# The products of the second down-projection, one behind each product of the first block's projections

## The reference

```python
def _attn_ref(q, k, v, tau):                       # q, k, v: 1 x 6016 x 256
    qn = q / (norm(q, axis=1) + 1e-06)
    kn = k / (norm(k, axis=1) + 1e-06)
    s = kn.transpose(0, 2, 1) @ qn / tau           # 256 x 256
    a = softmax(s)
    return v @ a

def _moe_ref(x, w_in, w_out, a, b):                # w_in 256 x 2048, w_out 2048 x 256
    h = x @ w_in
    P = a[0] + a[1] * h + a[2] * h**2 + a[3] * h**3
    Q = 1.0 + abs(b[0]) * abs(h) + abs(b[1]) * h**2
    return (P / (Q + 1e-06)) @ w_out

def _moe2_ref(x, w_in, w_out):
    h = x @ w_in
    return (h * clip(h + 3.0, 0.0, 6.0) / 6.0) @ w_out

out = _moe2_ref(_moe_ref(_attn_ref(q, k, v, tau)))
```

## Time and profile before

| | |
|---|---|
| median of 3 runs | 1137.36 us (1136.55 to 1137.97) |
| profiled execution, own time | 1137.52 us |
| its span | 1135.7 us |
| TensorE busy | 1111.2 us (98%) |
| VectorE, ScalarE, GpSimd busy | 889.9, 878.8, 781.0 us (78%, 77%, 69%) |
| matmuls | 6012 |
| mean granted clock of TensorE | 0.995 |

### The profile page before, as it was taken

How to read it: one execution, slowest core, us unless ns; L and a number is a source line. 1 busy time by engine, 2 the same in 40 slices (tenths; PEclk the granted TensorE clock), 3 DMA queues, 4 the chain that set the end, 5 groups by cost and what they waited for, 6 DMA issues and landing times.

```text
span 1135.7 us, 17913 instructions
## 1 busy us (share of the span) xinstructions
PE 1111.2 (98%) x6012; PEld 968.4 (85%) x6012; DVE 889.9 (78%) x1264; ACT 878.8 (77%) x1479; POOL 781.0 (69%) x625
## 2 busy tenths in 40 slices
PE   9988799999999999999999999999999999999998
PEld 8877588888888888888888888888888888888887
DVE  6699999987887887887887788787788788787722
ACT  6698888877877877877787787887787787787643
POOL 0278888776776776676676676677677677666643
PEclk9999899999999999999999999999999999999999
DMA  9931010010010010010010010010001000000000
GB/s 347 288 129 20 0 20 1 15 19 2 20 19 1 20 19 2 1 38 1 1 38 1 2 38 1 1 31 8 2 19 19 1 20 1 1 20 1 1 19 19
DMA packets 65729, 34.21 MB, mean 30 GB/s; under 512 B 47718, under 2 KB 58982, under 8 KB 65638
## 3 DMA queue, kind: packets, MB, share of 16 engines
q1 hardware_dynamic: 65072, 32.52, 10.1%
q10 hardware_dynamic: 566, 0.52, 0.1%
HBM read 26.87 MB, written 6.16 MB: 29 GB/s over the span
## 4 chain that ended last, share of the span: by engine, by line
PE 91%; DVE 5%; ACT 1%; issue 1%; DMA 0%; POOL 0%; SPq 0%; DVEq 0%; ACTq 0%
PE H L444 15%; PE H L445 14%; PE H L446 14%; PE OP L604 8%; PE OP L600 8%; PE OP L602 8%; PE YP L445 7%; PE YP L446 7%; PE YP L444 7%; PE OP L477 3%; DVE SQ L917 1%; DVE H L902 1%; DVE g_hi L910 1%; DVE T L895 1%; DMA qk<-in_k 0%
## 5 line engine op out<-in xcount | busy, mean ns | idle before, releaser
L398 POOL TENSOR_TENSOR SQ<-SQ,AB 128x512 f32<-128x512 f32 (+1 forms) x192 | 247.0, 1286 | 269.5 <-ACT SQ L700 269.3
L412 POOL TENSOR_TENSOR g_lo<-R,g_hi 128x512 fp32r<-128x512 f32 (+1 forms) x191 | 243.7, 1276 | 28.7 <-ACT g_hi L731 28.7
L404 POOL TENSOR_TENSOR g_lo<-SQ,Y 128x512 fp32r<-128x512 f32 (+1 forms) x192 | 244.9, 1275 | 6.2 <-DVE SQ L925 6.2
L698 ACT ACTIVATE AB<-H,absb 128x512 f32<-128x512 f32 (+1 forms) x192 | 130.4, 679 | 147.9 <-PE H L446 146.8
L600 PE MATMUL OP<-wd_hi,g_hi 128*128 128x256 f32 x748 | 210.0, 281 | 0.0
L604 PE MATMUL OP<-wd_hi,g_lo 128*128 128x256 f32 x748 | 210.0, 281 | 0.0
L602 PE MATMUL OP<-wd_lo,g_hi 128*128 128x256 f32 x748 | 209.8, 280 | 0.0
L895 DVE TENSOR_TENSOR T<-T,H 128x512 f32<-128x512 f32 (+1 forms) x192 | 129.3, 674 | 100.8 <-ACT T L706 100.8
L910 DVE SCALAR_TENSOR_TENSOR g_hi<-H,coef,Y 128x512 fp32r<-128x512 f32 (+1 forms) x192 | 141.7, 738 | 60.4 <-ACT Y L719 59.0
L444 PE MATMUL H<-vT_hi,wf_hi 128*128 128x512 f32 (+1 forms) x384 | 151.9, 396 | 13.6 <-DVE wf_lo L882 7.8
L917 DVE SCALAR_TENSOR_TENSOR SQ<-SQ,g_hi 128x512 f32<-128x512 f32 (+1 forms) x192 | 156.1, 813 | 6.6
(11 more groups left out here) (98 smaller groups left out, 2218.1 us busy)
## 6 DMA issues: line engine op xcount, KB each, us to landing
qk<-in_q SPq DMA_DIRECT2D x22, 256.0 KB, 5.4
qk<-in_k SPq DMA_DIRECT2D x22, 256.0 KB, 6.2
v_blocks<-in_v SPq DMA_DIRECT2D x88, 64.0 KB, 2.4
out<-o_tok SPq DMA_DIRECT2D x10, 512.0 KB, 2.8
wd_raw<-in_moe_w_out SPq DMA_DIRECT2D x8, 512.0 KB, 8.8
w_raw_a<-in_moe_w_in SPq DMA_DIRECT2D x2, 1024.0 KB, 11.6
wu_raw<-in_moe_w_in SPq DMA_DIRECT2D x4, 512.0 KB, 5.9
qk<-in_q SPq DMA_DIRECT2D x3, 128.0 KB, 2.8
```

The lines of the kernel that those rows point to most:

```text
L398: nc.gpsimd.tensor_tensor(SQ[:, j % 4, 0:w], SQ[:, j % 4, 0:w], AB[:, j % 2, 0:w], ALU.add)\
L404: nc.gpsimd.tensor_tensor(g1_lo[:, j % 4, 0:w], SQ[:, j % 4, 0:w], Y[:, j % 2, 0:w], ALU.mult)\
L412: nc.gpsimd.tensor_tensor(g2_lo[:, j % 4, 0:w], R[:, j % 2, 0:w], g2_hi[:, j % 4, 0:w].bitcast(fp32), ALU.subtract).then_inc(g2_lo_done, 1)
```

## The change

Down2 is cut into single products. `split_product` takes an optional `beside`, the chunk of down2 that belongs to the slot, and issues one of its matmuls behind each of its own three. `up1` passes numbers 0 to 5, `down1` numbers 6 to 11. The waits of down2 move with product 0, and `d2_done` is raised by the last one, number 11 (or 8 for the block of 384 tokens). Where a slot has no up1 or no down1, the six products of that half stand in a row in its place. Up2, all arithmetic, the number of matmuls and the code of the other engines stay as they are; `OUT_SLOT` too.

```diff
-            def split_product(psum, w_hi, w_lo, x_hi, x_lo, first, last):
+            def split_product(psum, w_hi, w_lo, x_hi, x_lo, first, last, beside=None, n=0):
                 nc.tensor.matmul(psum, w_hi, x_hi, start=first, stop=False)
+                if beside:
+                    down2_product(*beside, n)
                 nc.tensor.matmul(psum, w_hi, x_lo, start=False, stop=False)
-                return nc.tensor.matmul(psum, w_lo, x_hi, start=False, stop=last)
+                if beside:
+                    down2_product(*beside, n + 1)
+                done = nc.tensor.matmul(psum, w_lo, x_hi, start=False, stop=last)
+                if beside:
+                    down2_product(*beside, n + 2)
+                return done
...
+            def down2_product(blk, j, n):
+                tiles = width(blk) // P
+                if n >= 3 * tiles:
+                    return
+                if n == 0:
+                    wait_chunk(pe, g2_lo_done, (blk, j))
+                    if j == 0:
+                        if exists(blk - 1):
+                            pe.wait_ge(o_copied, blk)
...
+                i = n // 3
+                at = slice(i * P, (i + 1) * P)
+                gate = g2_lo if n % 3 == 2 else g2_hi
+                weight = wd2_lo if n % 3 == 1 else wd2_hi
+                done = nc.tensor.matmul(OP[:, i // 2, i % 2 * C:(i % 2 + 1) * C], gate[:, j % 4, at],
+                                        weight[:, j, :], start=j == 0 and i % 2 == 0 and n % 3 == 0,
+                                        stop=j == J - 1 and n % 3 == 2, skip_group_check=True)
+                if n == 3 * tiles - 1:
+                    done.then_inc(d2_done, 1)
+
+            def down2(blk, j, products):
+                for n in products:
+                    down2_product(blk, j, n)
...
                     if x := stage(t - 1, j - SHIFT2):
                         up2(*x)
-                    if x := stage(t - 1, j - SHIFT2 - LAG_DOWN2):
-                        down2(*x)
+                    x, y = stage(t - 1, j - SHIFT2 - LAG_DOWN2), stage(t, j - LAG_DOWN1)
                     if exists(t):
-                        up1(t, j, par)
+                        up1(t, j, par, x)
...
-                    if x := stage(t, j - LAG_DOWN1):
-                        down1(*x)
+                    elif x and last_chunk(*x):
+                        last_down2(*x)
+                    elif x:
+                        down2(*x, range(6))
+                    if y:
+                        down1(*y, x)
+                    elif x and not last_chunk(*x):
+                        down2(*x, range(6, 12))
```

More of the change, by code:

```diff
@@ L520, in fold, with up1 @@
                     done.then_inc(fold_made, 1)
-            def up1(t, j, par):
+            def up1(t, j, par, beside=None):
                 w = width(t)
@@ L531, in up1, with down1 @@
                     done = split_product(h1(t, j), wf_hi[:, c, cols], wf_lo[:, c, cols],
-                                         vT_hi[par][:, c, 0:w], vT_lo[par][:, c, 0:w], c == 0, c == CT - 1)
+                                         vT_hi[par][:, c, 0:w], vT_lo[par][:, c, 0:w], c == 0, c == CT - 1,
+                                         beside, 3 * c)
                 done.then_inc(u1_done, 1)
-            def down1(blk, j):
+            def down1(blk, j, beside=None):
                 w = width(blk)
@@ L544, in down1 @@
                                          wd1_lo[:, j, d * P:(d + 1) * P], g1_hi[:, j % 4, 0:w],
-                                         g1_lo[:, j % 4, 0:w], j == 0, j == J - 1)
+                                         g1_lo[:, j % 4, 0:w], j == 0, j == J - 1, beside, 3 * CT + 3 * d)
                 done.then_inc(d1_done, 1)
@@ L580, in last_down2 @@
                         done.then_inc(last_d2_done, 1)
[L582 to L606, removed]
@@ new lines, in down2_product @@
+            def down2_product(blk, j, n):
[7 more added lines that the diff above has]
+                            pe.wait_ge(o_copied, blk)
+                        if isinstance(blk, int) and blk == 0:
+                            pe.wait_ge(fold_lo, CT * len(PIECES))
+                    if isinstance(blk, int) and blk == 0 and j % 2 == 0:
+                        pe.wait_ge(wd2_lo_done, j // 2 + 1)
+                i = n // 3
[7 more added lines that the diff above has]
+                    done.then_inc(d2_done, 1)
```

## The result

The changed kernel takes 1171.87 us in the median of 5 runs (1170.38 to 1172.76), the kernel before 1137.1 (1136.55 to 1137.97): a ratio of 1.0304, 95% interval 1.0292 to 1.0316, so 34.8 us or 3.0% slower. The forecast was 1159.1, 21.6 us slower. Its own range of 1151 to 1169 missed the time by 3 us; the stated range of 1141 to 1178, widened for the rivals, held it.

The account below looks back on a forecast made before the run. TensorE's matmul rate was taken as the bound. Products 0, stalls 17.5 (steps 3 to 10), 1.3 (step 2), 0.95 (step 11), and step 1's 1.9 made 21.6 us: 1137.5 + 21.6 = 1159.1; own range 1151 to 1169, stated 1141 to 1178.

Parts of the forecast that it names:

- the stall: Up1 of slot 7 waits for rest(5), delayed through ACT's late copy: 2.19 us in each of steps 3 to 10.
- rival 2: TensorE slots: alternation costs, each change of bank and length stalling the array some 10 ns a pair; 20 us, 1179; 10%.
- rival 4: TensorE's clock falls in the stalls, each costing some 2 us more; 1177 us; 5%.
- theory A: The forecast's view: the copy on ACT is late, and what is queued behind it holds up1 of slot 7, 2.1 us.
- POOL's overlap with `product`: In rest(5)'s chain, POOL's quotient_lo moves by the same 2.3 us, so DVE's product still overlaps it at 1.47 us.
- slots 4 or 10: Up1 there keeps room in steps 3 to 11, 0.21 and 0.32 us, so no wait; waits would mean a misjudged ring.
- The products: TensorE's matmuls in 154 full slots: alternation itself costs 0 us, with bounds of -4.6 to +6.5 us.
- The toll of 13.3 ns for each product: Time per TensorE product beyond its columns, equal in three mixes of lengths, taken to be the same in alternation.
- Its picture: Short products in a row take 117.5 instead of 120 ns; the next long ones pay back the gain.
- where the forecast had 1.9: Step 1's term: 1.06 us in slot 6, 0.45 in slot 10, repeated in slot 0 of step 2; together 1.9 us.
- Rival 1: Short products' toll disappears beside long ones: 26.5 us saved, 1132.6; 5% for ending faster, 5% for a part.
- Rival 3: The stall is absorbed: the copy's lateness does not reach rest(5); 1139 to 1141 us; 5%.

Follow-up runs that it names:

- The first four experiments: Changed kernel with slot-5 row restored, 1145.24 us; with ACT's copy behind q_terms, 1146.7; with slot-7 row restored, 1151.33; kernel before with slot-5 row behind down1, 1143.11.
- the third experiment: Changed kernel, but in slot 7 of each step the 12 short products stand in a row ahead of up1; 1151.33 us.
- the first and second experiments: Changed kernel with slot 5's short products in a row ahead of up1, 1145.24 us; changed kernel with ACT's copy behind q_terms and p_start, 1146.7 us.
- the rows of three: Changed kernel with ACT's copy behind p_start, short products in threes behind each three long ones of up1 and down1; 1144.85 us.
- the short product ahead: Changed kernel with ACT's copy behind p_start, each short product ahead of its long one instead of behind; 1146.44 us.
- rows of six: Changed kernel with ACT's copy behind p_start, nothing alternating: up1, six short products, down1, six short products; 1146.34 us.
- the third and fourth experiments: Changed kernel with slot 7's short products in a row ahead of up1, 1151.33 us; kernel before with slot 5's row behind down1, 1143.11 us.

## Why the prediction was right, and what it mis-sized

The time lies in the stated range, but not by the stated sum. Of 34.8 us the forecast had 21.6; it had the stall right, and left out the falls of the clock and the toll of the new order. That the wider range held it is owed to the room given to rivals 2 and 4, both of which came in part.

**The stall: right in place, chain and size.** Forecast: copy 2.5 us too late, AB 2.34 late, up1 of slot 7 held for 2.08, first product 0.11 longer, in eight steps. Measured: 2.51, 2.31, 1.96 and 0.10. From the starts of up1, step 2 lost 1.2 us there (forecast 1.3) and step 11 0.8 (0.95). Together 8 x 2.06 + 2.0 = 18.5 against 19.75 in the forecast. The first four experiments take the chain apart, and each came out within 0.5 us of what theory A had given (1145, 1145 to 1147, 1151, 1143 to 1144). POOL's overlap with `product` moved along, as assumed (1.48 us). No wait came at slots 4 or 10 of steps 3 to 11.

**The clock: the step that failed.** The forecast took 2.1 us as too short for a fall and put that into rival 4 with 5%, reasoning from a wait of 1.6 us that had none. It fell behind five of the eight, 5 x 1.56 = 7.8 us. Rival 4 priced a fall at 2 us and let it come behind every stall, 18 us in all; less than half of that happened. The trace of before had a third long wait, of 2.3 us in the start-up, and the forecast did not read it. The first two lines below are from that trace, the last from that of the third experiment:

```profile
66.68 0.41 PE L444 MATMUL H<-vT_hi,wf_hi 128*128 128x384 f32 x1 [2.32 <-DVE wf_lo L882]
68.50:71.50 3.00, 3.00 (x9) 2.46 (x8) 2.67 (x6) 2.49 (x6) 1.83 (x3) 0.51 0.00 0
...
68.50:71.50 3.00, 3.00 (x18) 2.90 (x17) 2.66 (x5) 2.74 (x6) 1.83 (x3) 1.00 0.00 0
```

Behind this wait the clock fell, so 2.1 us stood between 1.6 without a fall and 2.3 with one. The same wait, 2.30 to 2.32 us long, stands in all eleven traces of this case. Behind it the clock fell in six (before, the changed kernel, the first and second experiments, the rows of three, the short product ahead) and stayed at 1.00 in five. So a wait of this length brings a fall in some executions and not in others, and 5% was too low for it.

The runs of the changed kernel say the same of slot 7: the mean granted clock is 0.990 and 0.991 in the two of 1170.4 and 1170.7 us, and 0.988 in the three of 1171.9 to 1172.8. Shorter waits had no fall. By the idle time that their rows give, where slot 7 has 1.79 us, these are 1.64 us in step 1 of the changed kernel (and of the seven experiments that have it), 0.91 in step 2 and 0.56 in step 11. What decides between equal waits stays open.

**The products: mis-sized, inside the bounds.** The toll of 13.3 ns for each product, taken from three mixes, does not hold for alternation. A slot takes 5.554, not 5.520 us: 154 x 34 ns = 5.2 us, where the forecast took 0 and had -4.6 to +6.5. Its picture, that a row of shorts gains 2.5 ns each and is paid back by the long ones behind, fits rows of six (27 ns more for a second row), not rows of three or single ones. What is shown is where the time goes: the pairs take 0.347 us, the old toll, and up2, six long products in a row, takes 1.39 instead of 1.36. Change of bank among short products, repeated stationary tiles and the position ahead or behind are ruled out; the cause of the 34, 27 and 20 ns is open.

**The rest.** 18.5 + 7.8 + 5.2 = 31.5 of 35.3 us. TensorE's waits without a releaser, at the two starts of the loop, went from 0.8 us in all to 1.7: 0.9 us that the forecast did not have. Most of what is left, 2.7 us, lies between slot 6 of step 1 and slot 6 of step 2, where the forecast had 1.9. Slot 6 of step 1 goes from 138.14 to 144.94, 6.80 us, instead of from 138.37 to 144.09, 5.72: 1.08 more, as forecast (1.06). Slot 10 and slot 0 of step 2 each cost about 0.3 us in place of 0.45. Slot 10 in the changed kernel:

```profile
160.50 0.34 PE L451 MATMUL H<-yT_hi,wu_lo 128*128 128x384 f32 x1
160.91 0.50 PE L445 MATMUL H<-vT_hi,wf_hi 128*128 128x512 f32 x1
```

Up1 wanted to start at 160.50 + 0.17 = 160.67 and is 0.24 us late, with 0.10 more in its first product. The other slots up to there take some 0.07 us more each (164.83 to 169.73 is 4.90 instead of 4.84), 0.9 us in all. The forecast put that at nothing: its bounds counted alternation only from slot 6 of step 2 on.

**Rivals.** Rival 1 falls: no product became cheaper, the pair of long and short takes 0.347 us, the old toll, and no variant in any order was below 5.520 us a slot. By the gap that the Trainium skill gives, "TensorE: Matmul & The Clock Gate", section "Back-to-back issue gap", 16.5 us would have come back (the forecast's estimate of 8.3 ns for each of 1992 short products); this case's traces do not bear it out. Rival 2 is right in sign at a quarter of its price (5.2 of 20 us), and the change of length that it names does not order the variants: four rows of three cost less than two of six. Rival 3 falls, since the lateness reaches `rest(5)` in full.

## What to carry to other kernels

Spreading an accumulation's last product over a longer stretch delays its "done" to the end of that stretch. Before doing it, look up who waits for that signal and, above all, what stands behind the waiting instruction in its engine's fixed order: here one copy, 1 us long and not itself urgent, cost some 25 us (falls of the clock included) because an urgent operation was queued behind it. Moving the copy behind that operation won 25.2 us back, and giving the last product its old place won 26.6. And moving work from ahead of a wait to behind it spends the room of that wait even where nothing waits yet; count the room (here 1.7 us against 1.4 + 2.3) before the move. And when a forecast hangs on what a wait does to the clock, read every wait of the trace that is near its length, those of the start-up too, and in more than one execution.

## What the hardware showed that was not expected

The granted clock of TensorE fell to 1.2 GHz behind waits of 2.0 us in the midst of an otherwise dense stream, five times of eight in one execution, and behind 2.5 us four times of eight. The same wait of 2.3 us in the start-up had a fall in six of eleven traces. The wait of 1.64 us in step 1, and those of 0.6 us in the third and fourth experiments, had none. A fall cost 1.56 us, beside 2.06 for the wait in front of it. And the order of the same 30 products changes their time: 5.520 us for one row of twelve short ones, 5.547 for two rows of six, 5.540 for four of three, 5.554 for twelve single ones, ahead or behind.
